# Attention scores in three blocks of 384 keys instead of two of 512 and one of 128, and a second buffer of output rows

## The chip, the cores and the metric

One core of a Trainium2 chip runs the whole program. The metric is the time of one execution on the device in microseconds (us). Below, TensorE is PE, VectorE is DVE, ScalarE is ACT, GpSimd is POOL, and SyncE, which issues most of the transfers, is SP.

## What is computed

Three layers follow each other: an attention, a mixture of experts that picks one expert per token, and a gated feed-forward layer. Only the attention is touched by the change. Its core is this, with batch 4, 8 heads, 1152 keys, heads of 64 and 576 queries (each the mean of two neighbouring rows of `q`):

```python
q_pool = q.reshape(B, H, S // 2, 2, D).mean(axis=3)
scores = np.matmul(q_pool, k.transpose(0, 1, 3, 2)) / np.sqrt(D)
scores = scores - np.max(scores, axis=-1, keepdims=True)
attn = np.exp(scores)
attn = attn / (np.sum(attn, axis=-1, keepdims=True) + 1e-09)
return np.matmul(attn, v)
# then: x = rows of tokens; moe picks e = argmax(x @ w_gate) and scales
#       relu(x @ w1[e]) @ w2[e]; last (silu(x @ w_gate) * (x @ w_val)) @ w_out
```

## The kernel before

The 32 heads are worked off in 16 pairs. In a pair each head has 576 queries: four tiles of 128 rows, and 64 rows that are left over. So a pair has nine tiles of query rows: tiles 0 to 3 of the first head, 4 to 7 of the second, and tile 8 with the left-over rows of both. For each tile a row of 1152 scores must be there before its maximum is known, and with it the exponentials.

All values are fp32; for precision the kernel splits operands into a high and a low part. A score tile is the sum of two matmuls (tile 8: of four) per block of keys. The row of 1152 keys was cut as 512 + 512 + 128:

- Two halves of 512 keys go to the PSUM banks `ps_s0` to `ps_s2`, taken in turn (`scores`, L785 to L792). Each half fills a bank.
- The last 128 keys of four tiles at once go to one further bank, `ps_r` (`scores_rem`, L805).
- DVE takes the maximum of each half (`largest_half`, L578) and, for four tiles at once, of the rests (`largest_rest`, L586), and then the negated maximum over the three (`neg_max`, L591).
- ACT computes the exponentials into `probs`, each with the sum of its row: `exp_half` (L538) and `exp_rem` (L521).
- PE turns the probabilities by 128x128 blocks into `ps_t` (`fill`, L694), ACT copies them to `p_hi` (L514), DVE takes the rest to `p_lo` (L657), and PE multiplies both with the values into `ps_o` (`products`, L761, and L770 for tile 8).
- The products of a head are copied out by DVE (`o_sb`, L598 and L601), PE turns them back (L725), and DVE scales them into the output rows `x_out` (L643, and L608 with L613 for tile 8). SP stores `x_out` to memory (`store`, L309 and L313).
- For the pair that follows, PE turns keys and queries in four groups (units "g"), ACT and DVE write high and low parts (`kept_rows`), and SP copies these to `kq_t`.

Three engines run the same list `UNITS` of 27 steps per pair, each in its own fixed order: "a" and "b" are the nine key chunks of the first and the second head, "c" tile 8 in three pieces, "g" the groups of the next pair, "x" the two turns of the results. "b" of one pair is worked off at the start of the body after it. At unit n PE fills one of the three buffers `ps_t` (which the unit three back must have left: `TR = 3`), and multiplies the unit three back (`LAG = 3`). The tables `SCORES_AT`, `MAXIMA_AT` and `EXP_AT` say behind which unit PE computes a tile's scores, DVE its maxima and ACT its exponentials; tile 0 in them is that of the next pair. A unit may have several of them. The first body ("first"), the last one ("last") and what is left after it ("tail") have only some of the units. Semaphores hold the engines to each other: `exp_done` says that a bank of scores is free, `t_free` that a `ps_t` is, `o_free` that `ps_o` is.

Of the kernel before, what the change touches and what calls it, by code (L numbers as in the profile page):

```python
# [8 lines left out]
ALU = mybir.AluOpType  # L9
# [3 lines left out]
P = 128  # L13
# [4 lines left out]
X_STORES = 3 * 16 + 1  # L18
# [4 lines left out]
class Shared:  # L23
# [3 lines left out]
    def __init__(self, nc, ctx, x_dram, experts, slot_tiles, ident, kept):  # L27
# [21 lines left out]
        self.x_out = sb("x_out", [P, 9 * 64])  # L49
        self.x_stored = ctx.enter_context(nc.semaphore("x_stored"))  # L50
# [11 lines left out]
def attention(nc, q, k, v, w_gate, w_out_gate, w1, x_dram, xs_dram, ys_dram, shared):  # L62
# [27 lines left out]
    MAIN = 8 * P  # L90
# [14 lines left out]
    SR = 3  # L105
# [9 lines left out]
    ]  # L115
    SCORES_AT = [(26, 26), (2, 2), (4, 5), (7, 8), (12, 13), (17, 17), (19, 20), (21, 22), (23, 24)]
    MAXIMA_AT = [(25, 25), (2, 2), (3, 4), (7, 8), (12, 13), (16, 16), (18, 19), (20, 21), (22, 23)]
    EXP_AT = [(0, 2, 2), (4, 4, 4), (7, 8, 8), (11, 11, 13), (16, 16, 17), (18, 19, 20), (21, 21, 21), (22, 23, 23), (25, 25, 25)]
# [3 lines left out]
    assert HALF_SCALE == 0.25 and len(UNITS) % TR == 0 and 2 * TILES % SR == 0  # L122
# [50 lines left out]
    with ctx:  # L173
# [21 lines left out]
        x_out, x_stored = shared.x_out, shared.x_stored  # L195
# [9 lines left out]

        S = [ps(f"ps_s{i}", 512) for i in range(SR)]
        R = ps("ps_r", 512)
# [15 lines left out]
        r_ready = sem("r_ready")  # L223
        max_done = sem("max_done")
        bias_ready = sem("bias_ready")
        exp_rem_done = sem("exp_rem_done")
# [16 lines left out]
        assert X_DMAS * PAIRS + 1 == X_STORES and x_out.shape[1] == TILES * D  # L243
# [25 lines left out]
        with nc.Block() as block:  # L269

            @block.sync
            def _(sp):
# [29 lines left out]
                def store(p, kind):  # L302
# [8 lines left out]
                        x_out[:, 0:QT * P].rearrange("p (t c) -> p t c", t=QT)).then_inc(x_stored, 16)  # L311
                    for h in range(2):
                        sp.dma_start(x_rows[bass.ds(b, 1), QT * P:SQ, bass.ds(g, 1), h * D:h * D + D].rearrange(  # L313
                            "b p g c -> (b p) (g c)"),
                            x_out[h * REM:h * REM + REM, QT * P:QT * P + D]).then_inc(x_stored, 16)
# [32 lines left out]
                zero_rows(0, 1).then_inc(x_stored, 16)  # L348
                with sp.Fori(1, LAST - 3, 2) as p:
                    next_pair(p, 1, "mid")  # L350
                    store(p - 1, "mid")
                    zero_rows(2 * p - 1, 2).then_inc(rows_zeroed, 16)
                    next_pair(p + 1, 0, "mid")
                    store(p, "mid")
# [5 lines left out]
                store(LAST - 3, "mid")  # L360
# [11 lines left out]
                store(LAST - 2, "mid")  # L372
# [3 lines left out]
                sp.wait_ge(x_stored, 16 * (X_DMAS * (LAST - 1) + 1))  # L376
# [4 lines left out]
                store(LAST - 1, "last")  # L381
                store(LAST, "tail")
# [107 lines left out]
            def _(act):  # L490
# [26 lines left out]
                def exp_rem(p, par, tile):  # L517

                    r = (tile % QT) * P
                    to = tile * SK  # L520
                    nc.scalar.activation(probs[:, to + MAIN:to + SK], R[:, r:r + P], ACT.Exp,  # L521
                                         bias=neg_max[:, tile:tile + 1],
                                         accum_out=sums[par][:, sum_col(tile, 2)]).then_inc(exp_rem_done, 1)

                def exp_half(p, par, kind, tile, h):

                    if h == 0:
# [7 lines left out]
                        if kind != "first" and tile == TC:  # L535
                            act.wait_ge(t_filled, upto(p, kind, every, UNIT_LAST["c"]))
                    at = tile * SK + h * 512
                    nc.scalar.activation(probs[:, at:at + 512], S[(2 * tile + h) % SR][:, :], ACT.Exp,  # L538
                                         bias=neg_max[:, tile:tile + 1],
                                         accum_out=sums[par][:, sum_col(tile, h)]).then_inc(exp_done, 1)  # L540

                def body(p, par, kind):
                    j = 0
                    for n, step in enumerate(UNITS):
# [3 lines left out]
                        for tile in range(TILES):  # L548
                            if kind != "tail" and EXP_AT[tile][0] == n:
                                exp_half(p, par, kind, tile, 0)  # L550
                            if kind != "tail" and EXP_AT[tile][1] == n:
                                exp_rem(p, par, tile)
                            if kind != "tail" and EXP_AT[tile][2] == n:
                                exp_half(p, par, kind, tile, 1)
# [7 lines left out]
            def _(dve):  # L562
# [18 lines left out]
                def largest_rest(p, tile):  # L581

                    if tile % QT == 0:
                        dve.wait_ge(r_ready, 3 * p + tile // QT + 1)
                        w = 1 if tile == TC else QT
                        nc.vector.tensor_reduce(  # L586
                            maxima[:, 3 * tile:3 * (tile + w)].rearrange("p (t s) -> p t s", s=3)[:, :, 2],
                            R[:, 0:w * P].rearrange("p (t c) -> p t c", t=w), AX, ALU.max).then_inc(max_done, 1)

# [70 lines left out]
                def body(p, par, kind):  # L660
                    j = 0
                    for n, step in enumerate(UNITS):
                        if step in steps(kind):
                            take(p, par, kind, j, step)
                            if lagged(kind, j) in UNIT_LAST.values():
                                outputs(p, kind, lagged(kind, j)[0])
# [1177 lines left out]
```

## Time and profile before

| | |
|---|---|
| median of three runs | 1478.25 us (1476.42 to 1483.18) |
| the profiled execution | 1476.28 us, of which its span is 1474.5 us |
| attention | from the start to some 607 us |
| one pair in its steady stage | 35.47 us |
| PE busy in that stage | 35.07 of 35.47 us |
| DVE busy | 32.82 of 35.47 us |
| ACT busy | 28.90 of 35.47 us |
| granted TensorE clock | full (2.4 GHz) all through that stage |

A matmul's busy time overlaps with that of the next one, so what a matmul costs is read from the distance of the starts, not from its duration. The same holds for DVE and ACT, where one instruction begins a little before the one ahead of it has ended.

### The profile page before, as it was taken

How to read it: one execution, taken by the hardware profiler on the slowest of the kernel's cores; microseconds unless marked ns; L12 is line 12 of the kernel's file. 1: busy time of each engine (PE TensorE's matmuls, PEld its weight loads, DVE VectorE, ACT ScalarE, POOL GpSimd, SP SyncE). 2: the span in 40 equal slices, each digit the busy share in tenths (PEclk: the TensorE clock that was granted, in tenths of full speed). 3: DMA queues.
4: the chain of work that ended last, by engine and by line, in shares of the span. 5: the costliest groups of instructions: out<-in, count | busy, mean ns of one | idle time of the engine just before them, and what ended most of it. 6: DMA issues, size and time to landing. Idle time of an engine off the chain costs nothing. (4 is left out here: it accounts for less than half of the span.)

```text
span 1474.5 us, 24891 instructions
## 1 busy us (share of the span) xinstructions
PE 1377.8 (93%) x7733; PEld 1195.3 (81%) x7734; DVE 873.2 (59%) x1658; ACT 638.4 (43%) x1549; POOL 345.2 (23%) x241
## 2 busy tenths in 40 slices
PE   3999999999999999739978999998999999999998
PEld 2788888888888888537767787887999999999997
DVE  2899999999999998673443444445632323223232
ACT  2888888788888887532034102004411111111111
POOL 3122222222222220279179205022101010100000
PEclk9999999999999999969998999999999999999999
DMA  7566666666666764356256313114400000000000
GB/s 164 124 139 139 138 138 142 146 144 145 145 149 145 195 132 153 101 193 247 88 199 233 116 43 107 43 57 142 150 32 15 29 15 17 26 0 21 0 22 22
DMA packets 127931, 156.85 MB, mean 106 GB/s; under 512 B 47633, under 2 KB 86545, under 8 KB 125841
## 3 DMA queue, kind: packets, MB, share of 16 engines
q1 hardware_dynamic: 111968, 114.35, 30.8%
q10 hardware_dynamic: 12880, 31.99, 6.5%
q0 software_dynamic: 3040, 9.96, 2.0%
q8 instruction: 25, 0.41, 0.1%
q14 instruction: 18, 0.14, 0.0%
HBM read 87.33 MB, written 29.10 MB: 79 GB/s over the span
## 5 line engine op out<-in xcount | busy, mean ns | idle before, releaser
L514 ACT ACTIVATE p_hi<-ps_t 128x512 fp32r<-128x512 f32 (+1 forms) x336 | 194.3, 586 | 69.1 <-PE ps_t L694 64.7
L657 DVE TENSOR_TENSOR p_lo<-ps_t,p_hi 128x512 fp32r<-128x512 f32 (+1 forms) x336 | 216.9, 666 | 12.4 <-ACT p_hi L514 7.8
L578 DVE TENSOR_REDUCE maxima<-ps_s 128x1 f32<-128x512 f32 x288 | 193.7, 686 | 41.5 <-PE ps_s L792 37.7
L538 ACT ACTIVATE probs<-ps_s,neg_max 128x512 f32<-128x512 f32 x288 | 198.6, 690 | 44.1 <-DVE neg_max L591 43.9
L792 PE MATMUL ps_s<-kq_t 128*128 128x512 f32 x640 | 199.7, 414 | 13.6 <-DMA kq_t<-kept_rows 9.5
L694 PE MATMUL ps_t<-ident,probs 128*128 128x128 f32 x1296 | 198.5, 274 | 1.4 <-DVE kept_rows L569 0.8
L1026 POOL TENSOR_TENSOR w_parts<-raw_w,w_parts 128x1024 fp32r<-128x1024 f32 x64 | 150.9, 2396 | 184.5 <-ACT w_parts L1096 184.4
L694 PEld LDWEIGHTS ps_t<-ident,probs 128*128 128x128 f32 x1296 | 156.0, 140 | 46.3 <-DVE p_lo L657 9.6
L1642 ACT ACTIVATE silu<-ps_g 128x384 f32<-128x384 f32 x72 | 35.4, 491 | 314.6 <-PE ps_g L1748 314.6
L1695 DVE TENSOR_TENSOR silu<-ps_g,silu 128x384 f32<-128x384 f32 x72 | 40.1, 558 | 210.7 <-ACT silu L1642 210.7
L1096 ACT ACTIVATE w_parts<-raw_w 128x1024 fp32r<-128x1024 f32 x64 | 67.1, 1059 | 220.0 <-PE ps_h L1423 104.2
L761 PE MATMUL ps_o<-p_hi,v_hl 128*128 128x512 f32 x288 | 137.7, 478 | 8.4 <-DVE o_sb L598 5.2
L792 PEld LDWEIGHTS ps_s<-kq_t 128*128 128x128 f32 x640 | 114.7, 192 | 37.9 <-DMA kq_t<-kept_rows 9.9
L761 PE MATMUL ps_o<-p_lo,v_hl 128*128 128x512 f32 x288 | 113.6, 394 | 0.0
L1746 PE MATMUL ps_g<-mxt_hi,wg 128*128 128x384 f32 x288 | 97.5, 339 | 2.4 <-DVE mxt_lo L1670 2.4
L1748 PE MATMUL ps_g<-mxt_hi,wg 128*128 128x384 f32 x288 | 97.7, 339 | 0.0
L1747 PE MATMUL ps_g<-mxt_lo,wg 128*128 128x384 f32 x288 | 97.2, 338 | 0.0
L1421 PE MATMUL ps_h<-w_parts,xst_hi 128*128 x200 | 83.0, 415 | 14.6 <-POOL w_parts L1026 11.9
L1748 PE MATMUL ps_v<-mxt_hi,wv 128*128 128x384 f32 x288 | 96.4, 335 | 0.0
L1746 PE MATMUL ps_v<-mxt_hi,wv 128*128 128x384 f32 x288 | 96.4, 335 | 0.0
L1747 PE MATMUL ps_v<-mxt_lo,wv 128*128 128x384 f32 x288 | 96.4, 335 | 0.0
L1446 PE MATMUL ps_y<-w_parts,ht_hi 128*128 x200 | 81.7, 409 | 5.4 <-DVE ht_lo L1289 2.8
(190 smaller groups left out, 2786.5 us busy)
## 6 DMA issues: line engine op xcount, KB each, us to landing
raw_w<-in_moe_w ACTq DMA_DIRECT2D x61, 512.0 KB, 4.1
kq_t<-kept_rows SPq DMA_DIRECT2D x32, 608.0 KB, 6.2
kq_t<-kept_rows SPq DMA_DIRECT2D x32, 320.0 KB, 7.1
raw_k<-in_k SPq DMA_DIRECT2D x32, 288.0 KB, 5.7
raw_v<-in_v SPq DMA_DIRECT2D x16, 576.0 KB, 5.5
kq_t<-kept_rows SPq DMA_DIRECT2D x32, 288.0 KB, 6.5
raw_q<-in_q SPq DMA_DIRECT2D x32, 256.0 KB, 4.1
y_by_slot<-x_out SPq DMA_DIRECT2D x25, 256.0 KB, 2.0
```

The lines of the kernel that those rows point to most:

```text
L514: nc.scalar.activation(p_hi[prob_ring(kind, m)][:, 0:w], T[ring(kind, j)][:, 0:w], ACT.Copy).then_inc(hi_ready, 1)
L538: nc.scalar.activation(probs[:, at:at + 512], S[(2 * tile + h) % SR][:, :], ACT.Exp, bias=neg_max[:, tile:tile + 1], accum_out=sums[par][: ...
L578: nc.vector.reduce_max(maxima[:, 3 * tile + h:3 * tile + h + 1], S[(2 * tile + h) % SR][:, :], AX).then_inc(max_done, 1)
L657: nc.vector.tensor_tensor(p_lo[n][:, 0:w], t[:, 0:w], p_hi[n][:, 0:w].bitcast(F32), ALU.subtract).then_inc(t_free, 1)
L694: last = nc.tensor.transpose(dst[:, n * P:(n + 1) * P], src, ident[:, :])
L761: last = nc.tensor.matmul(O[:, :], v_hl[v_par][:, c * P:(c + 1) * P], part[:, :], start=(i == 0 and n == 0), stop=(i == CH - 1 and n == 1))
L792: last = nc.tensor.matmul(S[(2 * tile + h) % SR][:, :], w, kq_t[par][:, at:at + 512], start=(n == 0), stop=(n == len(ops) - 1))
L1026: nc.gpsimd.tensor_tensor(w_part(n, parity, 1, at, PIECE), raw[j % RAW][:, :], w_part(n, parity, 0, at, PIECE).bitcast(F32), ALU.subtract) ...
L1421: nc.tensor.matmul(HB[h][:, :], xh, dyn(0, base, 0, at), start=(c == 0), stop=False)
L1746: nc.tensor.matmul(dst, wh, xh, start=(c == 0), stop=False)
L1747: nc.tensor.matmul(dst, wh, xl, start=False, stop=False)
L1748: last = nc.tensor.matmul(dst, wl, xh, start=False, stop=(c == DC - 1))
```

## The change

A score row is cut in three blocks of 384 keys. All blocks use the four PSUM banks that scores had together: block 0 goes to `ps_s0` and `ps_s3` in turn, block 1 always to `ps_s1`, block 2 to `ps_s2`. `ps_r`, its semaphores, `scores_rem`, `exp_rem` and `largest_rest` are gone. ACT takes the blocks of a tile in the order 1, 2, 0. The list `UNITS` and the tables of places have other entries (now three per tile). There are two buffers `x_out`, each with a semaphore of its own for its stores, and SP waits for both where it waited for one.

```diff
-    SCORES_AT = [(26, 26), (2, 2), (4, 5), (7, 8), (12, 13), (17, 17), ...
+    SCORES_AT = [(25, 26, 26), (2, 2, 2), (4, 5, 5), (6, 7, 7), (8, 12, 12), (12, 14, 15), ...
+    EXP_ORDER = (1, 2, 0)
...
-        S = [ps(f"ps_s{i}", 512) for i in range(SR)]
-        R = ps("ps_r", 512)
+        S = [ps(f"ps_s{i}", 512) for i in range(4)]
...
+        def bank(par, tile, b):
+            return S[b if b else 3 * ((par + tile) % 2)][:, 0:BLK]
...
-                    at = tile * SK + h * 512
-                    nc.scalar.activation(probs[:, at:at + 512], S[(2 * tile + h) % SR][:, :], ACT.Exp,
+                    at = tile * SK + b * BLK
+                    nc.scalar.activation(probs[:, at:at + BLK], bank(par, tile, b), ACT.Exp,
                                          bias=neg_max[:, tile:tile + 1],
-                                         accum_out=sums[par][:, sum_col(tile, h)]).then_inc(exp_done, 1)
+                                         accum_out=sums[par][:, sum_col(tile, b)]).then_inc(exp_done, 1)
...
-                def largest_half(p, tile, h):
-
-                    dve.wait_ge(s_ready, 2 * TILES * p + 2 * tile + h + 1)
-                    nc.vector.reduce_max(maxima[:, 3 * tile + h:3 * tile + h + 1],
-                                         S[(2 * tile + h) % SR][:, :], AX).then_inc(max_done, 1)
+                def largest(p, par, tile, b):
+
+                    dve.wait_ge(s_ready, 3 * (TILES * p + tile) + b + 1)
+                    nc.vector.reduce_max(maxima[:, 3 * tile + b:3 * tile + b + 1], bank(par, tile, b), AX
+                                         ).then_inc(max_done, 1)
+                    if b == 2:
+
+                        dve.wait_ge(max_done, 3 * (TILES * p + tile + 1))
+                        nc.vector.tensor_reduce(neg_max[:, tile:tile + 1], maxima[:, 3 * tile:3 * tile + 3], AX,
+                                                ALU.max, negate=True).then_inc(bias_ready, 1)
...
-                    dve.wait_ge(x_stored, 16 * (X_DMAS * (p - 1) + 1))
+                    dve.wait_ge(x_stored[1 - par], 8 * X_DMAS * (p - 1 - (1 - par)) + 16)
...
-                        pe.wait_ge(exp_done, 2 * TILES * p + 2 * tile + h - SR + 1)
+                        pe.wait_ge(exp_done, 3 * (TILES * p + tile - 1) + b)
...
-                        at = head * HEAD + h * 512
-                        last = nc.tensor.matmul(S[(2 * tile + h) % SR][:, :], w, kq_t[par][:, at:at + 512],
+                        at = head * HEAD + b * BLK
+                        last = nc.tensor.matmul(bank(par, tile, b), w, kq_t[par][:, at:at + BLK],
                                                 start=(n == 0), stop=(n == len(ops) - 1))
```

How the instructions stand now is seen best in the middle of a pair, where the last "b" products, the pieces of tile 8 ("c") and the groups of the next pair ("g") meet the scores of tile 4. First PE, before. `ps_t<-ident,probs` is a turn of probabilities (x3: a "c" piece), `ps_t<-ident,raw_k` one of keys (a "g" group), `ps_s` are scores of 512 keys, `ps_r` the rests of four tiles, ISA and REGISTER_ALU are waits and counters.

```order
L694 MATMUL ps_t<-ident,probs 128x128 x3
L785 REGISTER_ALU
L788 ISA
L792 MATMUL ps_s<-kq_t 128x512 x2
L706 REGISTER_ALU
L694 MATMUL ps_t<-ident,probs 128x128 x3
L785 REGISTER_ALU
L792 MATMUL ps_s<-kq_t 128x512 x2
L800 ISA
L805 MATMUL ps_r<-kq_t 128x128 x8
L706 REGISTER_ALU
L694 MATMUL ps_t<-ident,raw_k 128x128
```

And PE after the change; the scores here are blocks 1 and 2 of tile 4 and block 0 of tile 5, the products in rows 2 and 3 those of the last "b" chunk.

```order
L677 MATMUL ps_t<-ident,probs 128x128 x3
L744 MATMUL ps_o<-p_hi,v_hl 128x512
L744 MATMUL ps_o<-p_lo,v_hl 128x512
L677 MATMUL ps_t<-ident,raw_k 128x128 x4
L769 REGISTER_ALU
L776 MATMUL ps_s<-kq_t 128x384 x2
L769 REGISTER_ALU
L776 MATMUL ps_s<-kq_t 128x384 x2
L769 ISA
L776 MATMUL ps_s<-kq_t 128x384 x2
L689 REGISTER_ALU
L677 MATMUL ps_t<-ident,probs 128x128 x3
```

The eight matmuls on the rests are gone, the two score groups of 512 keys that stood one behind each "c" piece have become three of 384 in a row, and the group "g" 1, which stood ahead of the "c" pieces, now stands between the second and the third.

Then DVE at the same place, before: the copy of the second head's products (`o_sb`), the low parts of the "c" pieces, the maxima of both halves and of the rests, and the negated maximum.

```order
L601 COPY o_sb<-ps_o 128x512
L656 REGISTER_ALU
L657 TENSOR_TENSOR p_lo<-ps_t,p_hi 128x384
L577 REGISTER_ALU
L578 TENSOR_REDUCE maxima<-ps_s 128x1
L657 TENSOR_TENSOR p_lo<-ps_t,p_hi 128x384
L577 REGISTER_ALU
L578 TENSOR_REDUCE maxima<-ps_s 128x1
L584 ISA
L586 TENSOR_REDUCE maxima<-ps_r 128x4
L590 REGISTER_ALU
L591 TENSOR_REDUCE neg_max<-maxima 128x1
```

And DVE after the change.

```order
L643 TENSOR_TENSOR p_lo<-ps_t,p_hi 128x384
L587 COPY o_sb<-ps_o 128x512
L571 REGISTER_ALU
L572 TENSOR_REDUCE maxima<-ps_s 128x1
L571 REGISTER_ALU
L572 TENSOR_REDUCE maxima<-ps_s 128x1
L576 ISA
L577 TENSOR_REDUCE neg_max<-maxima 128x1
L571 REGISTER_ALU
L572 TENSOR_REDUCE maxima<-ps_s 128x1
L635 REGISTER_ALU
L563 SCALAR_TENSOR_TENSOR kept_rows<-ps_t,kept_rows 128x512
```

Behind the copy now stand two reductions of 384 (blocks 1 and 2 of tile 4), the negated maximum and block 0 of tile 5, with no low part between them; the low part of the third "c" piece comes after a `kept_rows`.

## Rows read from the trace of the kernel before

**Rows 1.** The page: the span, and the TensorE clock granted in 40 slices.

```profile
span 1474.5 us, 24891 instructions
...
PEclk9999999999999999969998999999999999999999
```

**Rows 2.** Busy us of PE, PEld, DVE, ACT, POOL; clock; DMA: thirteen pairs, one pair.

```profile
83.62:544.76 461.14, 455.97 (x2927) 387.97 (x2926) 427.03 (x872) 375.96 (x1028) 96.10 (x79) 1.00 0.63 146
331.92:367.39 35.47, 35.07 (x226) 29.85 (x225) 32.82 (x68) 28.90 (x80) 7.38 (x6) 1.00 0.63 143
```

**Rows 3.** Timeline of PE, one steady pair: start, duration, engine, line, what, [idle before].

```profile
340.05 1.09 PE L792 MATMUL ps_s<-kq_t 128*128 128x512 f32 x4
340.98 1.01 PE L805 MATMUL ps_r<-kq_t 128*128 128x128 f32 x8
341.82 0.62 PE L694 MATMUL ps_t<-ident,probs 128*128 128x128 f32 x4
342.20 0.48 PE L761 MATMUL ps_o<-p_hi,v_hl 128*128 128x512 f32 x1
```

**Rows 4.** Timeline of PE, last stage: its matmuls of 384 columns.

```profile
1154.69 0.33 PE L1746 MATMUL ps_g<-mxt_hi,wg 128*128 128x384 f32 x1
...
1158.87 0.39 PE L1761 MATMUL ps_out<-wo,a_hi 128*128 128x512 f32 x1
```

**Rows 5.** Timeline of PE, same pair: three places where it stands.

```profile
345.49 0.60 PE L694 MATMUL ps_t<-ident,probs 128*128 128x128 f32 x4
346.35 0.50 PE L761 MATMUL ps_o<-p_hi,v_hl 128*128 128x512 f32 x1 [0.26 <-DVE o_sb L598]
...
346.92 0.60 PE L694 MATMUL ps_t<-ident,probs 128*128 128x128 f32 x4
347.27 0.48 PE L761 MATMUL ps_o<-p_hi,v_hl 128*128 128x512 f32 x1
...
363.21 0.60 PE L694 MATMUL ps_t<-ident,probs 128*128 128x128 f32 x4
363.92 0.47 PE L761 MATMUL ps_o<-p_hi,v_hl 128*128 128x512 f32 x1
...
365.27 0.71 PE L792 MATMUL ps_s<-kq_t 128*128 128x512 f32 x2
365.98 0.66 PE L694 MATMUL ps_t<-ident,probs 128*128 128x128 f32 x4
```

**Rows 6.** Timeline of DVE, same pair: its reductions and what follows.

```profile
338.64 0.28 DVE L586 TENSOR_REDUCE maxima<-ps_r 128x1 f32<-128x128 f32 x1
...
340.71 1.29 DVE L578 TENSOR_REDUCE maxima<-ps_s 128x1 f32<-128x512 f32 x2 [0.41 <-PE ps_s L792]
342.02 0.69 DVE L586 TENSOR_REDUCE maxima<-ps_r 128x4 f32<-128x512 f32 x1
342.75 0.16 DVE L591 TENSOR_REDUCE neg_max<-maxima 128x1 f32<-128x3 f32 x1
...
358.03 0.55 DVE L657 TENSOR_TENSOR p_lo<-ps_t,p_hi 128x384 fp32r<-128x384 f32 x1
358.49 0.68 DVE L578 TENSOR_REDUCE maxima<-ps_s 128x1 f32<-128x512 f32 x1
```

**Rows 7.** Groups by form: busy us, mean ns, idle before: the exponentials on ACT.

```profile
L538 ACT ACTIVATE probs<-ps_s,neg_max 128x512 f32<-128x512 f32 x288 | 198.6, 690 | 44.1 <-DVE neg_max L591 43.9
...
L521 ACT ACTIVATE probs<-ps_r,neg_max 128x128 f32<-128x128 f32 x144 | 52.6, 365 | 0.0
```

**Rows 8.** Timeline of all engines, the opening: an exponential on ACT.

```profile
31.06 0.69 ACT L538 ACTIVATE probs<-ps_s,neg_max 128x512 f32<-128x512 f32 x1 [1.21 <-DVE neg_max L591]
```

**Rows 9.** Timeline of the SP queue, same pair: copies and stores.

```profile
363.86 2.59 SPq L299 DMA_DIRECT2D kq_t<-kept_rows  x1
...
380.79 1.33 SPq L313 DMA_DIRECT2D x_rows<-x_out  x2
```

**Rows 10.** The page, transfers: the copies of 320 KB, us to landing.

```profile
kq_t<-kept_rows SPq DMA_DIRECT2D x32, 320.0 KB, 7.1
```

More of the change, by code:

```diff
@@ L48, in __init__ @@
         self.raw_loaded = [ctx.enter_context(nc.semaphore(f"raw_w_loaded{i}")) for i in range(RAW)]
-        self.x_out = sb("x_out", [P, 9 * 64])
-        self.x_stored = ctx.enter_context(nc.semaphore("x_stored"))
+        self.x_out = sb("x_out1", [P, 9 * 64])
+        self.x_stored = [ctx.enter_context(nc.semaphore(f"x_stored{i}")) for i in range(2)]
         self.x_dram = x_dram
@@ L242, in attention @@
         KQ_DMAS, X_DMAS, COPIES = 6, 3, 3
[L243 removed]
+        assert X_DMAS * PAIRS // 2 + 1 == X_STORES and x_out[0].shape[1] == TILES * D
+        def bank(par, tile, b):
+            return S[b if b else 3 * ((par + tile) % 2)][:, 0:BLK]
         def sum_col(tile, part):
@@ L515, in take, with exps @@
                                          ).then_inc(hi_ready, 1)
[L517 to L527, printed above, removed]
+                def exps(p, par, kind, tile, b):
+                    if b == EXP_ORDER[0]:
                         act.wait_ge(bias_ready, TILES * p + tile + 1)
@@ L548, in body @@
                         for tile in range(TILES):
[L549 to L554, printed above, removed]
+                            for at, b in zip(EXP_AT[tile], EXP_ORDER):
+                                if kind != "tail" and at == n:
+                                    exps(p, par, kind, tile, b)
                 for g in range(GROUPS):
@@ L684, in _ @@
                     group_lo(g, g % TR)
-                largest_half(0, 0, 0)
-                largest_half(0, 0, 1)
-                largest_rest(0, 0)
+                for b in range(3):
+                    largest(0, 0, 0, b)
                 over_pairs(dve, body)
@@ L708, in fill @@
                     if what in "ab":
-                        done = 2 * TILES * p + (2 * QT if what == "a" else -2)
+                        done = 3 * (TILES * p + (QT if what == "a" else -1))
                         pe.wait_ge(exp_done, done)
@@ L779, in operands, with scores @@
                             for h in heads for part in range(2)]
-                def scores(p, par, tile, h, opening=False):
-                    if not (opening and 2 * tile + h < SR):
-                        pe.wait_ge(exp_done, 2 * TILES * p + 2 * tile + h - SR + 1)
-                    if tile in (0, QT) and h == 0:
+                def scores(p, par, tile, b, opening=False):
+                    if not (opening and (tile == 0 or (tile == 1 and b == 0))):
+                        pe.wait_ge(exp_done, 3 * (TILES * p + tile - 1) + b)
+                    if tile in (0, QT) and b == 0:
                         pe.wait_ge(kq_copied[tile // QT], 16 * COPIES * (p + 1))
@@ L822, in body @@
                             opening = kind == "first" and tile > 0
-                            if SCORES_AT[tile][0] == n:
-                                scores(*of, tile, 0, opening)
-                            if SCORES_AT[tile][1] == n:
-                                scores(*of, tile, 1, opening)
-                                if tile % QT == 0:
-                                    scores_rem(*of, tile, opening)
+                            for b in range(3):
+                                if SCORES_AT[tile][b] == n:
+                                    scores(*of, tile, b, opening)
                     if kind == "tail":
@@ L841, in _ @@
                     group(g, T[g % TR]).then_inc(t_filled, 1)
-                scores(0, 0, 0, 0, True)
-                scores(0, 0, 0, 1, True)
-                scores_rem(0, 0, 0, True)
+                for b in range(3):
+                    scores(0, 0, 0, b, True)
                 over_pairs(pe, body)
@@ L992, in _ @@
             def _(sp):
-                sp.wait_ge(shared.x_stored, 16 * X_STORES)
+                for i in range(2):
+                    sp.wait_ge(shared.x_stored[i], 16 * X_STORES)
                 for i in range(X_EARLY, len(X_LOADS)):
```

86 lines of the change are left out of this document (32 added, 54 removed), and 4 rows, old and new, of the table UNITS.

## The prediction

> **What bounds the kernel now.** I began with the page for the share of each engine and the granted clock. The clock is at its upper level (2.4 GHz) in nearly all slices of the attention [rows 1]; nothing in the change makes PE idle for long, so I price all of the steady stage at that level. Then I put the busy times of the engines side by side over thirteen pairs, each counted from the second turn of the results to the same turn of the next pair. The reader is to see that 461.14 / 13 = 35.47 us go to a pair, that PE is busy for 455.97 / 461.14 = 99% of it, DVE for 93% and ACT for 82% [rows 2]. So PE sets the pace, DVE is close behind (2.65 us free in a pair) and ACT is not in question.
>
> Busy time hides small stands of PE, since matmuls are pipelined. In the timeline I compared each group with the same group elsewhere. Four turns followed by products take 347.27 - 346.92 = 0.35 us from start to start; once in a pair they take 346.35 - 345.49 = 0.86, where the first products into `ps_o` wait for DVE's copy out of it, and once 363.92 - 363.21 = 0.71, where the same bank waits for tile 8's results [rows 5]. Two score matmuls, which by the price below take 0.465, take 365.98 - 365.27 = 0.71 before a turn that needs its `ps_t` [rows 5]. With three lesser ones that I found by the same comparison (some 0.3 together, an estimate) PE stands 0.50 + 0.36 + 0.25 + 0.3 = 1.4 us in a pair. Its own work is then 35.47 - 1.4 = 34.07.
>
> **The change on PE, which carries the forecast.** In a pair PE does 40 matmuls of 512 columns and 20 of 128 for scores: two parts by two halves for eight tiles, four by two for tile 8, and the rests likewise. Afterwards it is two parts by three blocks for eight tiles and four by three for tile 8, so 60 of 384. The count stays 60, and so do the columns (40 x 512 + 20 x 128 = 60 x 384 = 23,040). What changes is the price per matmul:
> - 512 columns: four take 340.98 - 340.05 = 0.93, or 0.2325 each [rows 3].
> - 128 columns: eight take 341.82 - 340.98 = 0.84, or 0.105 each [rows 3].
> - 384 columns: none in this stage, but the last stage runs 24 of them, with the same operand types, in 1158.87 - 1154.69 = 4.18, or 0.174 each [rows 4].
>
> The line through 384 and 512 would give a matmul of 128 columns 0.174 - 2 x 0.0585 = 0.057. It costs 0.105. These 20 short ones are what the change gets rid of: 40 x 0.2325 + 20 x 0.105 = 11.40 before, 60 x 0.174 = 10.44 after, 0.96 less in a pair. A group of turns right behind the short ones takes 342.20 - 341.82 = 0.38 [rows 3] instead of 0.35 [rows 5], three times in a pair, and the new order has one change fewer from turns to other matmuls (26 runs of turns in a pair against 27; each costs its successor some 0.08, by the same comparison of groups). Together 0.1 more. PE's own work becomes 34.07 - 1.06 = 33.0 us.
>
> The Trainium skill (TensorE: Matmul & The Clock Gate, section Back-to-back issue gap) says that in a stream of weight loads and matmuls the sustained spacing is some 81 ns at 128 columns and 131 ns at 512. By that the 60 matmuls cost 6.9 us before and, on the line between, 6.9 after: no gain at all. The trace does not agree (232.5 and 105 ns here), so I give it a small chance below.
>
> **DVE.** A reduction of 512 takes 0.68 to 0.69, one of 128 takes 0.28 [rows 6], so 384 should take 0.28 + 0.40 x 2/3 = 0.55, and being pipelined it holds the engine for about as long as the low part of 384 columns does, 358.49 - 358.03 = 0.46 [rows 6]. Two of 512 in a row last 1.29 together and one alone 0.69, so one holds it for 0.60 when something independent follows; it holds it for 0.73 when the negated maximum must wait for its end (342.75 - 342.02) [rows 6]. Per pair, before: 12 at 0.60, 6 at 0.73, 2 rests of four tiles at 0.73, one of 128 at 0.28 + 0.04: 13.4. After: 18 at 0.465 and 9 at 0.465 + 0.13 = 0.595: 13.7. The negated maxima stay. So DVE gets 0.3 to 0.4 us more, and needs 32.82 + 0.35 = 33.2 us of a pair if it never waits. That is a second floor, as high as PE's. It also caps the gain at 35.47 - 33.2 = 2.3 us a pair.
>
> The Trainium skill (VectorE: DVE Perf Modes, section on the TRN2 errata) warns that each instruction pays a fixed cost and advises tiles of 512 elements or more; with its 120 + N cycles for a PSUM source the reductions would cost 0.75 us more a pair instead of 0.35. The trace has a fixed part as well (0.28 for 128 against 0.68 for 512), and most of it is hidden by the instruction ahead.
>
> **ACT.** The exponentials take 690 ns for 512 and 365 ns for 128 [rows 7]; on that line 384 takes 365 + 325 x 2/3 = 582, and 3 x 582 = 1746 against 2 x 690 + 365 = 1745 per tile. Nothing changes, and each tile still has three.
>
> **Waits.** Blocks 1 and 2 now have one bank each. A tile's block 2 can be computed only when ACT is done with the last tile's blocks 1 and 2, and only then come its maximum, the negated maximum and the next exponentials. With nothing between, a round is two exponentials (1.15), two matmuls and their latency (0.35 + 0.3), a reduction (0.58) and the negated maximum (0.2): 2.6 us, nine rounds 23.4 of a pair of 34. So it has slack of a third, and the tables put one to two units (0.9 us each) between. I followed the new order unit by unit with the spacings above. The stand at the first copy of `ps_o` nearly goes: PE has six scores (1.04) ahead of it instead of four (0.93), and tile 0's maxima end some 0.4 earlier on DVE. A new one of some 0.3 arises behind the place shown for DVE, where the copy (0.60), three reductions and a negated maximum (1.7) and a `kept_rows` (0.65) stand before the buffer of "g" 1 is free; the wait for tile 8's results grows from 0.35 to about 0.5; single waits for an exponential give 0.2. That comes to 1.0 to 1.1. A count misses small latencies, and DVE has less room than before, so I take the old sum of 1.4. Bounds: 0.9 at the least (33.9 us a pair), and at the most what turns the gain round, below.
>
> **What stays at nothing.** The second `x_out` takes a wait from DVE that does not bind: the stores of the pair are issued from 380.79 to 382.1 [rows 9], and the next writer of `x_out` comes behind the "c" pieces, at 358.03 + 35.47 = 393.5 [rows 6]. SP's copies for the next pair come one unit earlier, and tile 0's scores one unit earlier too: the last copy for them is issued at 363.86 [rows 9] and lands 7.1 later [rows 10], at 371.0; its reader came at 340.05 + 35.47 = 375.5 [rows 3], and 3 us or so remain. In the opening, tiles follow each other bound by the round above (ACT stands 1.21 per tile for the negated maximum [rows 8]); a tile should take the same time, for one exponential more in the round (0.5) and shorter matmuls and reductions (0.25 and 0.15 less). I take 0, with -1.5 to +1.5.
>
> **The sum.** A pair takes 33.0 + 1.4 = 34.4 instead of 35.47, 1.07 less. It counts for the thirteen pairs of [rows 2], the one before and the one after them: 15 x 1.07 = 16 us. Nothing behind the attention changes. The profiled execution took 1476.3 and would take 1460; the median of the runs shown is 2 above it, and goes to 1462.
>
> **The rivals.**
> - *DVE takes over and eats the gain* (0.20). For it: DVE's floor of 33.2 is above PE's. Against: it still has 1.2 us free in a pair of 34.4. If it keeps most of its idle time (2.0 of 2.65), a pair takes 35.2 and the kernel 1474; with all of it 35.85 and 1484.
> - *Slower, by the single banks* (0.12). The round decides: if at each tile PE's turns and products fall between exponential and scores, so that a round costs 2.6 + 1.8 (two units) = 4.4 at half of the tiles and 3.5 at the others, a pair takes 35.5, and with a third unit at five tiles 37, 1.5 more: 1478 + 23 = 1501. It decides from 3.94 per round (35.47 / 9) on. Against it: block 0 has two banks and can be filled early, and the tables place exponentials ahead of the scores that need them.
> - *No gain on PE* (0.03). If 384 columns cost here 0.19 instead of 0.174, the 0.96 is gone and the kernel stays at 1478. Rows of 384 columns speak against it.
> - *More than forecast* (0.07). The stands fall to 0.9 or below: 15 x 1.6 = 24 less, 1454 or lower.
> - The forecast, 34.1 to 34.7 a pair, has the rest (0.58): 1457 to 1466.
>
> **How the numbers follow.** A difference of 0.5% (7 us) is about what a measurement can tell from none. Faster by more: 0.58 + 0.07 and a quarter of DVE's case, 0.70. Within: the rest of DVE's case and the one without gain, 0.18. Slower: 0.12. The range runs from 1453 to 1478 and leaves out the slower case and little below.
>
> **What would show it.** Right: a pair of about 34.4 in the timeline of PE, its score matmuls 0.174 apart, DVE's reductions 0.55 long and 27 in a pair, DVE's share at 96 to 97%, the 0.50 stand at the first copy mostly gone, the time behind the attention as before. Wrong: score matmuls further apart than 0.18, PE waiting in its scores for `probs` (the bank of ACT), or waits of PE for `p_lo` that come to more than 2 us a pair.

## The result and the profile after

The change makes the kernel slower: 1520.37 us (median of four runs, 1518.82 to 1521.09) against 1478.09 us for the kernel before in the same comparison, a ratio of 1.0273 with a 95% interval of 1.0253 to 1.0292. The forecast was 1462 us and its range ended at 1478, so it has the wrong sign. Each ratio below is likewise against runs of the kernel before that were made beside the runs of the edit (medians 1480.12, 1482.87 and 1481.55 us).

The page of the changed kernel answers to [rows 1]: the span is 44.8 us longer, and the mean granted clock is down to 0.8 in two slices of the attention, where it was 0.9 or more before. The last row counts the packets of a queue that fetches instructions; on the page of the kernel before it had 18 packets and 0.14 MB.

```profile
span 1519.3 us, 25250 instructions
...
PEclk9998989999999999995998999999999999999999
...
q14 instruction: 48, 0.39, 0.1%
```

The windows answer to [rows 2]; columns as there. The first is the opening up to the second turn of the results, the second the thirteen pairs behind it, the third the rest. The last two are neighbouring pairs.

```profile
0.00:82.38 82.38, 56.47 (x302) 48.09 (x304) 49.12 (x108) 45.74 (x127) 21.44 (x29) 1.00 0.60 134
82.38:590.95 508.57, 465.06 (x2926) 407.69 (x2926) 429.98 (x950) 371.11 (x1028) 95.65 (x79) 0.95 0.58 133
590.95:1519.30 928.35, 863.52 (x4508) 764.33 (x4507) 397.99 (x698) 216.43 (x396) 227.39 (x135) 0.97 0.26 84
162.18:196.84 34.66, 34.46 (x227) 30.56 (x227) 33.07 (x74) 28.56 (x80) 7.41 (x7) 1.00 0.62 147
196.84:241.44 44.60, 37.56 (x227) 32.52 (x227) 33.11 (x74) 28.64 (x80) 7.32 (x7) 0.89 0.50 115
```

The thirteen pairs take 508.57 instead of 461.14, 47.4 more; the opening takes 1.2 less and all that follows 1.4 less (928.35 against 1474.5 - 544.76 = 929.74). So the whole loss lies in the steady stage, and there in every second pair. Counted from second turn to second turn the pairs last 34.67, 45.13, 34.66, 44.60, 34.66, 44.21, 34.68, 44.04, 34.66, 43.99, 34.68, 43.90, 34.69. Seven are short, 0.80 below the 35.47 of before; six are long, by 9.64 above the short ones on the mean. 6 x 9.64 - 13 x 0.80 = 47.4: the sum closes.

The long ones have a hole on DVE. This is DVE's timeline around the first of them (start, duration, engine, line, what; in brackets the idle time before it and what ended it).

```profile
126.67 1.64 DVE L572 TENSOR_REDUCE maxima<-ps_s 128x1 f32<-128x384 f32 x3
128.34 0.16 DVE L577 TENSOR_REDUCE neg_max<-maxima 128x1 f32<-128x3 f32 x1
128.44 0.69 DVE L643 TENSOR_TENSOR p_lo<-ps_t,p_hi 128x512 fp32r<-128x512 f32 x1
137.30 1.89 DVE L643 TENSOR_TENSOR p_lo<-ps_t,p_hi 128x512 fp32r<-128x512 f32 x3 [8.17 <-issue]
```

DVE ends its work at 129.1 and starts the next instruction at 137.3. It isn't kept by another engine: "issue" says that it waited for nothing that the profile shows. When it comes back it does three low parts in a row that had piled up. The place is always the same. DVE's fixed order runs in a loop whose body (`over_pairs`, L265) is two pairs long, the first "mid" body with parity 1 and the second with parity 0, and the hole is where the end of that body meets its beginning. Seven rounds have six jumps back, and there are six holes. The waits of the attention (engine, line, what for: us in total, times, longest) show who hangs on them:

```profile
ACT p_hi L519 <- PE ps_t L677: 102.3, 121, 7.5
DVE p_lo L643 <- issue: 49.3, 6, 8.3
...
PE ps_t L677 <- DVE p_lo L643: 36.4, 6, 6.1
```

PE's timeline at the same place:

```profile
130.40 1.64 PE L776 MATMUL ps_s<-kq_t 128*128 128x384 f32 x6
138.05 1.11 PE L677 MATMUL ps_t<-ident,probs 128*128 128x128 f32 x4 [6.00 <-DVE p_lo L643]
139.84 0.80 PE L744 MATMUL ps_o<-p_hi,v_hl 128*128 128x512 f32 x1 [0.68 <-DVE o_sb L584]
...
143.21 1.05 PE L677 MATMUL ps_t<-ident,probs 128*128 128x128 f32 x4
143.91 0.78 PE L744 MATMUL ps_o<-p_hi,v_hl 128*128 128x512 f32 x1
```

PE's next turns need a `ps_t` that DVE has not left (`t_free`), so PE stands for 6.0 us and then for another 0.68. The granted clock fell while PE stood, and PE resumes at the lower level (1.2 GHz): four turns take 143.91 - 143.21 = 0.70 from start to start where they take 0.35 in [rows 5]. The windows show the clock (the number before the last two) at 0.50 and then back at 1.00:

```profile
135.30:138.00 2.70, 0.00 (x0) 0.00 (x0) 0.70 (x2) 0.00 (x0) 0.59 (x2) 0.50 0.52 188
138.05:145.50 7.45, 6.77 (x22) 5.60 (x23) 5.17 (x10) 3.48 (x9) 0.00 (x0) 0.50 0.00 1
145.60:150.00 4.40, 4.40 (x29) 3.89 (x28) 4.18 (x10) 3.21 (x9) 0.00 (x0) 1.00 0.00 0
```

In the pair from 196.84 the mean granted clock is 0.89, and 9.94 us are lost on a hole of some 8: the hole is paid once as waiting and then again in slow matmuls.

Where there is no hole, the kernel does about what the prediction said. PE in the short pair:

```profile
163.88 0.60 PE L677 MATMUL ps_t<-ident,probs 128*128 128x128 f32 x4
164.54 0.61 PE L776 MATMUL ps_s<-kq_t 128*128 128x384 f32 x2
...
168.29 1.55 PE L776 MATMUL ps_s<-kq_t 128*128 128x384 f32 x8
169.69 0.60 PE L677 MATMUL ps_t<-ident,probs 128*128 128x128 f32 x4
...
175.34 1.64 PE L776 MATMUL ps_s<-kq_t 128*128 128x384 f32 x6
176.81 0.60 PE L677 MATMUL ps_t<-ident,probs 128*128 128x128 f32 x4
```

Eight score matmuls take 169.69 - 168.29 = 1.40, or 0.175 each. Two stands are to be seen: 164.54 - 163.88 = 0.66 for four turns, 0.31 over their 0.35, and 176.81 - 175.34 = 1.47 for six scores, 0.42 over 6 x 0.175. PE's weight loads (PEld) name the cause of both, a bank of scores that ACT has not left:

```profile
164.54 0.30 PEld L776 LDWEIGHTS ps_s<-kq_t 128*128 128x128 f32 x2 [0.30 <-ACT probs L535]
...
176.36 0.30 PEld L776 LDWEIGHTS ps_s<-kq_t 128*128 128x128 f32 x2 [0.47 <-ACT probs L535]
```

And from the page, the reductions and the exponentials of 384:

```profile
L535 ACT ACTIVATE probs<-ps_s,neg_max 128x384 f32<-128x384 f32 x432 | 247.8, 580 | 52.3 <-DVE neg_max L577 52.3
...
L572 DVE TENSOR_REDUCE maxima<-ps_s 128x1 f32<-128x384 f32 x432 | 228.7, 550 | 34.9 <-PE ps_s L776 28.4
```

### The profile page after: what moved, and what is told of

Its sections match the earlier page's. It is cut to its first block and busy times, and to the rows that moved or that the text cites. A ratio compares the mean times of both kernels' runs of the same rounds, so it can differ in the third digit from the quotient of the medians.

```text
span 1519.3 us, 25250 instructions
## 1 busy us (share of the span) xinstructions
PE 1385.1 (91%) x7733; PEld 1220.1 (80%) x7734; DVE 877.1 (58%) x1754; ACT 633.3 (42%) x1549; POOL 344.5 (23%) x241
## 5 line engine op out<-in xcount | busy, mean ns | idle before, releaser
L535 ACT ACTIVATE probs<-ps_s,neg_max 128x384 f32<-128x384 f32 x432 | 247.8, 580 | 52.3 <-DVE neg_max L577 52.3
L776 PE MATMUL ps_s<-kq_t 128*128 128x384 f32 x960 | 237.0, 360 | 17.5 <-DMA kq_t<-kept_rows 9.4
L572 DVE TENSOR_REDUCE maxima<-ps_s 128x1 f32<-128x384 f32 x432 | 228.7, 550 | 34.9 <-PE ps_s L776 28.4
L677 PE MATMUL ps_t<-ident,probs 128*128 128x128 f32 x1296 | 203.3, 279 | 36.9 <-DVE p_lo L643 36.8
L677 PEld LDWEIGHTS ps_t<-ident,probs 128*128 128x128 f32 x1296 | 165.5, 144 | 61.9 <-DVE p_lo L643 39.3
L776 PEld LDWEIGHTS ps_s<-kq_t 128*128 128x128 f32 x960 | 170.5, 195 | 53.3 <-ACT probs L535 20.9
L1610 ACT ACTIVATE silu<-ps_g 128x384 f32<-128x384 f32 x72 | 35.4, 492 | 313.9 <-PE ps_g L1716 313.9
L744 PE MATMUL ps_o<-p_hi,v_hl 128*128 128x512 f32 x288 | 141.6, 492 | 6.7 <-DVE o_sb L584 5.2
L744 PE MATMUL ps_o<-p_lo,v_hl 128*128 128x512 f32 x288 | 116.7, 405 | 0.0
L409 POOL TENSOR_TENSOR v_hl<-raw_v,zeros 128x1152 fp32r<-128x1152 f32 x16 | 42.3, 2647 | 236.2 <-PE ps_o L753 236.0
```

The costliest lines, as they stand in the source:

```text
L535: nc.scalar.activation(probs[:, at:at + BLK], bank(par, tile, b), ACT.Exp, bias=neg_max[:, tile:tile + 1], accum_out=sums[par][:, sum_col( ...
L572: nc.vector.reduce_max(maxima[:, 3 * tile + b:3 * tile + b + 1], bank(par, tile, b), AX).then_inc(max_done, 1)
L677: last = nc.tensor.transpose(dst[:, n * P:(n + 1) * P], src, ident[:, :])
L744: last = nc.tensor.matmul(O[:, :], v_hl[v_par][:, c * P:(c + 1) * P], part[:, :], start=(i == 0 and n == 0), stop=(i == CH - 1 and n == 1))
L776: last = nc.tensor.matmul(bank(par, tile, b), w, kq_t[par][:, at:at + BLK], start=(n == 0), stop=(n == len(ops) - 1))
```

## The experiments

The theory that the two traces suggest: DVE's loop body has grown by the split of the rows (nine tiles with three reductions each instead of two, two pairs in a body, and a counter or wait for most of them; the four-tile rests are gone), and no longer stays in what DVE keeps of its code, so that each jump back has to fetch it. The trace records 249 of DVE's instructions per round before and 282 after: 12 reductions and 21 counters and waits more. The expectations below count 281, one less, which changes none of what follows from it. The rivals: the second buffer of output rows, and the banks with their new order.

**The loop alone.** DVE's bodies are written out one after the other, with nothing else changed, so that DVE never jumps back.

```diff
-                over_pairs(dve, body)
+                body(0, 0, "first")
+                for q in range(1, LAST, 2):
+                    body(q, 1, "mid")
+                    body(q + 1, 0, "mid")
+                # then "last" and "tail" as before
```

> The changed kernel with DVE's loop over the pairs written out: the same DVE work in the same order, but as one straight line of instructions with no jump back and no register arithmetic for the waits. In the changed kernel every second pair takes 44 to 45 us instead of 34.67, and in each of these DVE stands 8.2 us right behind the end of its loop body, with nothing released that it waits for. Theory F (fetch): DVE's instructions are no longer at hand when it jumps back. Then the six stands of 8.2 us go, every pair takes about 34.6 us, and the kernel takes 1520 - 6 x 9.5 = 1463 us. Theory W (waits): the stand comes from the order of the work (the alternating bank of block 0 or the alternating output buffer, which also have a period of two pairs). Then it stays, and the kernel takes 1515 to 1520.

Measured: 1466.93 us, ratio 0.9914 (0.9886 to 0.9942). No stand on DVE for issue above 0.3 us is left in the steady stage, and the pairs take 34.5 and 34.7 in turn. DVE does the same work in the same order; the jump and the register arithmetic for the waits have gone, and 53 us with them. The next runs part the two.

**The same loop at another place.** The loop is kept, and an argument of it sets at which instruction, counted within the blocks of code, DVE's body begins.

```diff
-            with eng.Fori(1, LAST, 2) as p:
+            with nc.Fori(1, LAST, 2, engines=[eng.engine],
+                         head_slot={mybir.EngineType.DVE: 0}) as p:
```

> The changed kernel, with the first instruction of DVE's loop body placed at the start (slot 0) of a block of 256 instructions; the loop and all work are as they were. Theory F in its form by position (the body must lie in two such blocks; 281 instructions from slot 0 do): the stands go, 1463 us. Theory F in its form by length (a body of more than 256 instructions never stays, 249 before did and 281 does not): nothing changes, 1520. Theory W: 1520.

Measured: 1470.96 us, ratio 0.9939 (0.9912 to 0.9966); the stands went as expected, but the kernel is 8 us above the 1463 expected. Its thirteen pairs (columns as above) and its instruction packets:

```profile
85.22:537.69 452.47, 449.23 (x2926) 397.13 (x2926) 429.98 (x950) 371.22 (x1028) 95.82 (x79) 1.00 0.64 149
```

```profile
q14 instruction: 19, 0.16, 0.0%
```

With 236 in place of the 0:

> As the run before, but the body starts at slot 236, so that its 281 instructions end in a third block (236 + 281 = 517). Theory F by position: the stands are there as in the changed kernel, 1515 to 1525 us. By length: 1520. Theory W: 1520. It tells something only together with the run before.

Measured: 1504.27 us, ratio 1.0174 (1.0149 to 1.02). The pair with the jump takes 40.4 to 41.4, and the stand is there again, but at 4.6 us instead of 8.2, so that the kernel stays below the 1515 to 1525 expected:

```profile
DVE p_lo L644 <- issue: 27.5, 6, 4.6
```

```profile
q14 instruction: 49, 0.40, 0.1%
```

One kernel, with nothing but its place in the code moved, is 33 us slower or faster, with the jump and all its arithmetic in both. What is fetched is seen as well: 30 packets more, five for each of the six jumps. They come round by round: in the changed kernel two fall into the stand from 208.9 to 217.1 and three into the rest of that round, while the kernel before has not one between 140 and 555 us.

**One buffer of output rows**, everything else as changed.

```diff
-        x_out, x_stored = [sb("x_out0", [P, TILES * D]), shared.x_out], shared.x_stored
+        x_out, x_stored = [shared.x_out, shared.x_out], shared.x_stored
...
-                    dve.wait_ge(x_stored[1 - par], 8 * X_DMAS * (p - 1 - (1 - par)) + 16)
+                    if not (isinstance(p, int) and p == 1):
+                        dve.wait_ge(x_stored[par], 8 * X_DMAS * (p - par) + 16)
```

> The changed kernel with a single buffer of output rows again (its two semaphores and the loop kept; DVE waits for the stores of the pair before). Theory F: the loop body has 282 instructions instead of 281, the stands stay, 1520 us. Theory W with the alternating output buffer as its cause: every pair is like the other, near 34.7 us, and the kernel near 1465.

Measured: 1528.06 us, ratio 1.0331 (1.0298 to 1.0364). The six stands are there (49.5 us in total), the short pairs take 34.76. The second buffer is not what costs. Without it the kernel is rather some 0.6% slower still, of which 0.1 us is seen in each short pair; 4.7 of the 6.3 us between the two spans lie behind the thirteen pairs, a stretch that takes 928 to 937 us in the fourteen traces whatever was changed. The prediction had put this buffer at nothing.

**How much is held.** Two more places, 228 and 108.

> The changed kernel with DVE's loop body at slot 228, eight slots ahead of the run at 236: its 281 instructions then end at 228 + 281 = 509 and lie in two blocks of 256. Theory F by position (two blocks are held): no stands, near the run at slot 0 (1471 us). If what counts is something finer (blocks of 128, or the place of the loop's end), the stands are there: 1500 us or more.

Measured at 228: 1470.61 us, ratio 0.992 (0.9903 to 0.9937), 18 packets, no stand.

> The changed kernel with DVE's body at slot 108: 108 + 281 = 389, two blocks of 256, but four of 128 (0 to 127 up to 384 to 511). At slots 0 and 228 it lay in three blocks of 128, at 236 in four. If what is held are blocks of 256, two of them: no stands, 1471 us. If it is three blocks of 128: stands, 1500 us or more.

Measured at 108: 1505.55 us, ratio 1.0165 (1.0133 to 1.0198):

```profile
DVE p_lo L644 <- issue: 27.2, 6, 4.6
```

```profile
q14 instruction: 50, 0.41, 0.1%
```

A packet is 8 KB (0.41 MB in 50). The Trainium skill (Runtime: NRT & Kernel Launch, section Instruction fetch mechanics) says that 256 instructions are 16 KiB, by which a packet would be 128 instructions (an estimate). Counted in blocks of 128, the body of 282 lies in three from 0 (to 282) and from 228 (to 510, blocks 128 to 511), and in four from 236 (to 518) and from 108 (to 390). In blocks of 256 it lies in two from 0, 228 and 108 and in three from 236. Only the first count sorts the four times rightly: three blocks of 128 without a stand, four with one. The Trainium skill's two lines of 256 would have spared the body at 108, and it isn't spared. By the same count a body of 249 can never lie in more than three, wherever it begins (127 + 249 = 376, under 384), and one of 282 lies in four if it begins at 103 to 127 of a block (236 and 108 are both at 108 of one). That the old body of 249 is spared everywhere is this count's word; the old kernel was not run with its start at 236 and nothing else changed.

**Why 8.2 us at one place and 4.6 at the others.** DVE's register instructions are in the trace too, and they show that the changed kernel waits twice. The first instruction of the body (a register operation of L265) comes 4.5 to 4.7 us after the jump, and the second another 4.0 to 4.1 after it, at each of the six jumps. At 236 and 108 there is one wait of 4.9 to 5.1, and the second instruction follows within 0.1; at 0 and 228 the first comes after 0.2 to 0.3. So in the changed kernel the first instruction seems to lie alone at the end of its block (slot 127 of 128), and the next is in a block that must be fetched as well. From 127 the body reaches 409, which is four blocks, as the count asks. The run with one output buffer has the same pair of waits.

**The old kernel with a body of the new length.** 32 memsets of one element each (0.06 us each) are added to DVE's body, which makes 249 + 32 = 281 instructions (282 in the trace, with a register move), and the body begins at 236. Blocks, banks, tables and buffer are those of before.

```diff
+        spare = sb("spare", [P, 32])
...
+                    if kind == "mid" and what in "ab":
+                        if i < 8:
+                            k = 16 * par + 8 * (what == "b") + i
+                            nc.vector.memset(spare[0:1, k:k + 1], 0.0)
```

> The kernel before with 32 tiny writes of one element in DVE's loop (16 a pair), so that its body has 281 instructions like the changed one, and with the body at slot 236. Scores, order and buffers are those of before. Theory F: six stands on DVE at the loop's end as in the changed kernel at slot 236, some 5.9 us a loop; with 1 us a pair at the most for the writes the kernel takes 1478 + 36 + 0 to 15 = 1514 to 1529 us. Theory W (the new order or the new banks): no stands, 1478 to 1493.

Measured: 1522.37 us, ratio 1.0273 (1.0252 to 1.0294): the kernel before loses 40 us with none of the change in it. That the ratio is the changed kernel's own is chance: it has the shorter stands (4.6 against 8.2 us) and not the gain of the short pairs. Two neighbouring pairs, the wait and the packets:

```profile
162.32:197.79 35.47, 35.08 (x227) 29.83 (x225) 32.96 (x84) 28.89 (x80) 7.38 (x6) 1.00 0.62 143
197.79:240.36 42.57, 38.00 (x227) 31.88 (x225) 33.02 (x84) 29.02 (x80) 7.37 (x6) 0.92 0.53 120
```

```profile
DVE spare L642 <- issue: 26.8, 6, 4.7
```

```profile
q14 instruction: 48, 0.39, 0.1%
```

The pair without the jump is at the old 35.47 to the hundredth, so the memsets themselves cost nothing. The pairs with it take 41.2 to 42.8. Length and start were changed together here.

And the kernel before with DVE's bodies written out (the edit of the first experiment):

> The kernel before with DVE's loop written out, as in the first run for the changed one. It had no stands at the loop's end, so the gain is only that of the register arithmetic of the waits: 0 to 5 us, 1474 to 1480. If the score blocks are what makes the changed one faster when it is written out (35.47 against 34.6 a pair), this stays some 12 us above it.

Measured: 1480.27 us, ratio 0.9976 (0.996 to 0.9991), pairs of 35.18. The kernel before loses nothing like this at its jumps. Against the changed kernel written out in the same way (0.9914, pairs of 34.5 and 34.7) it stays 0.6% above: that is what the change gains where no jump is in the way.

**A hint at the jump.** The loop is told to announce its jump back, on DVE; first with the body where the changed kernel has it, then at 236.

```diff
+            with nc.Fori(1, LAST, 2, engines=[eng.engine], hint_back_edge=True) as p:
```

Measured: 1470.84 us, ratio 0.9923 (0.9905 to 0.9941); 18 packets.

> The changed kernel with DVE's body at slot 236, where it had stands of 4.6 us, and with the hint that names the jump. The hint at the old place left only 18 packets on the queue for instructions, as if nothing had been fetched anew. If the hint makes DVE keep or fetch in time what it needs, no stands: 1471 us, and the packets tell which (18: kept, some 48: fetched ahead). If the hint only shifted the body to a good place there, the stands of the run at 236 are back: 1504.

Measured: 1469.81 us, ratio 0.9908 (0.9877 to 0.9938); 20 packets, pairs of 34.67 and 34.96, no stand. The hint mends both places. But it does so in a way that I did not expect: I had thought that the blocks would still be fetched, only in time, with 48 packets. They aren't fetched again, and that at 236 too, where the body lies in four blocks. So what is held cannot be simply "three blocks and no more"; the place and the hint both decide it. One reading would fit every count here: there is room for four blocks, and without a hint DVE also fetches the block behind the one that it is in, so that a body in four blocks needs a fifth (five packets in each round), one in three needs four (none), and the hint puts the jump's target in place of the block behind (none). No run tests this reading, and how the hint works stays open.

**The blocks without the new order.** Blocks of 384, their banks and both buffers, with the list `UNITS` and the places of before (blocks 1 and 2 where the second half stood or next to it), DVE's body at 0.

> Blocks of 384 keys, four banks and two output buffers as in the changed kernel, DVE's loop body at slot 0, but the units and the places of scores, maxima and exponentials as in the kernel before (block 0 where the first half stood, block 1 where the second stood or with it, block 2 with the second). It parts the price of the matmuls from the order. If the price is what gains: PE's own work in a pair is again 33.1 us, and with stands of 1.6 to 2.2 a pair takes 34.7 to 35.3, the kernel 1470 to 1479. If the order is what gains, a pair takes 35.4 or more, the kernel 1480 or more.

Measured: 1494.89 us, ratio 1.0087 (1.0057 to 1.0118). The second of the two cases expected came true (35.4 or more, 1480 or more). With these banks the price of the matmuls alone brings no gain, as thirteen pairs show, and the waits for the banks:

```profile
88.50:559.44 470.94, 457.11 (x2927) 394.70 (x2927) 434.69 (x950) 375.62 (x1028) 96.27 (x85) 1.00 0.62 143
```

```profile
PEld ps_s L777 <- ACT probs L536: 24.1, 52, 0.8
...
PE ps_s L777 <- ACT probs L536: 7.7, 20, 0.5
```

A pair takes 36.23, 0.75 more than before. Four times in each of thirteen pairs PE's weight load waits for ACT to be done with a bank of scores; with the new order and the body at 0 the row over its thirteen pairs reads `11.0, 33, 0.5`. So the new order is worth 470.94 - 452.47 = 18.5 us in thirteen pairs, 1.42 a pair, and is what makes the single banks bearable.

**The fastest.** DVE's and ACT's bodies both written out, the edit of the first experiment twice.

> The changed kernel with the loops of DVE and ACT written out, the candidate for the fastest. A pair took 34.51 and 34.70 us in turn with DVE's alone. ACT is busy for some 29 us of it, so its register arithmetic can cost only where PE waits for an exponential: 0 to 0.2 us a pair less, 1464 to 1467 where the first run had 1467.

Measured: 1462.49 us, ratio 0.9864 (0.9837 to 0.9891): this version is faster than both kernels, by 1.4% against the kernel before.

```profile
80.93:526.59 445.66, 444.08 (x2927) 398.18 (x2927) 425.32 (x950) 370.41 (x1028) 95.85 (x79) 1.00 0.65 152
```

A pair takes 34.28 (445.66 / 13), 1.19 less than before. That is 0.33 less than with DVE's loop alone written out (450.00 / 13 = 34.62), where 0 to 0.2 was expected. ACT's jump and its register arithmetic are worth that together; they were not parted.

## Why the prediction was wrong

**The step that failed** is its first paragraph: "nothing in the change makes PE idle for long, so I price all of the steady stage at that level", and with it the part on DVE, which counted what the reductions last ("DVE gets 0.3 to 0.4 us more") and never how many instructions the body of the loop has. That number went from 249 to 282, and the body began where 282 instructions don't stay. What the runs showed in place of a PE that never idles: DVE stands 8.2 us behind each of six jumps, PE stands 6.0 of them and then works on at 1.2 GHz. The same kernel with the body at 0 takes 452.47 us for the thirteen pairs instead of 508.57, so the stands cost 56.1 us, which no term of the sum and none of the rivals held. The one slower rival had another mechanism, and the range left it out. Undoing the stands in five ways (written out, two places, a hint at the own place and at 236) gives ratios of 0.991 to 0.994, and bringing length and place into the kernel before gives 1.0273. The growth alone does not cost (starts at 0 and 228): it takes the length and the start together.

The Trainium skill (Runtime: NRT & Kernel Launch, section Instruction fetch mechanics) warns that a taken branch whose target lies outside a window of two pages stalls the engine until the page is there. The trace agrees that there is such a stall, 8.2 us for each jump of the changed kernel. It could have been a rival, with the instructions counted in the two programs. It would not have been a firm one: the Trainium skill gives no price for it, and its window of 512 instructions holds 282 as well as 249, unless the body begins badly.

**PE's own work** was right: 0.174 per matmul of 384 columns forecast, 0.175 measured, in place of 0.2325 and 0.105. The doubt from the Trainium skill's spacing figures was rightly given little: the 60 matmuls of 384 take 60 x 0.175 = 10.5 us here, not the 6.9 estimated from them. One addition in the term is loose: 3 x 0.03 for the turns behind the short matmuls and 0.08 for the change fewer make 0.17, where 0.1 was taken.

**The stands** were mis-sized. I took 1.4 us a pair; the short pair takes 34.66, so the 33.0 of work forecast leave 1.65 (1.7 with the 0.17 above), where the count by hand had said 1.0 to 1.1. The stand of 0.50 at the first copy of `ps_o` has gone, as forecast. But where I had put 0.2 for single waits for an exponential there are 0.31 and 0.42, at the two places shown above: the single banks took back the larger part of what that stand had cost. The short pair gained 0.80 instead of 1.07.

**Every second pair** takes 0.3 more than the other even where nothing is fetched (34.67 and 34.96 with the body at 228 or at 0), while all pairs of the kernel before take 35.45 to 35.50. With that the mean gain is 0.66 a pair, 8.7 us in thirteen (461.14 - 452.47), and the kernel comes to some 1471 us rather than 1462. DVE's jump is the lesser part of it: with its loop written out 0.2 is left (34.5 and 34.7), and with ACT's written out too it is still 0.13 to 0.21. The bank of block 0 and the output buffer alternate from pair to pair as well; neither was tried in a kernel without stands, so the cause of the rest stays open.

**DVE and ACT.** 550 and 580 ns per block, forecast 0.55 us and 582 ns. DVE is busy for 33.07 of a short pair (forecast 33.2 of 34.4): it did not take over.

**The single banks** were a rival at 0.12, with 35.5 to 37 us a pair. With the old order it came out at 36.23. With the new one and the body at 0, PE's weight loads wait 11.0 us for them in thirteen pairs, 0.85 a pair. The rival's mechanism is real and the tables hold it off. Its upper price was too low by its own terms: a third unit of 0.9 us at five tiles adds 4.5 us to 35.5, not 1.5.

**The opening and the rest**: -1.2 us (forecast 0, with 1.5 either way) and -1.4, the latter well within what this stretch differs by from trace to trace (928 to 937 us). **The second buffer** was put at nothing, and is worth 0.1 us in a short pair.

## What to carry to other kernels

Where an engine's work runs in a loop, count the instructions of the body on each engine, counters and waits included, before and after a change, as one counts bytes for a buffer: past the point at which the code is held, every round pays microseconds, however little the added instructions last (shown here for DVE). Whether it pays depends on where the body begins, so an edit ahead of a loop can also bring or take such a stand; six "issue" stands at one line and more packets on the instruction queue are its mark. And a stand on an engine off the critical path is priced with the slow matmuls that follow it.

## What the hardware showed that I had not expected

- A jump back cost DVE 8.2 us for each round in the changed kernel and 4.6 us with the body at 236 or at 108, with the same 30 packets more. The first is two waits, of 4.6 us before the body's first instruction and of 4.1 before its second; the other is one.
- Without a hint a body that lies in three blocks of 8 KB by the count above fetched nothing at its jumps, and one in four was fetched anew in every round (four places and one padded body); with a hint nothing was fetched again at either place tried.
- After a stand of 6 us PE ran at 1.2 GHz from 138.05 to 145.5. The groups from there to 145.90 take 7.85 us; at the starts of full clock they would take 3.75 (a turn group 0.35, a pair of products 0.55, a score matmul 0.175). By this estimate some 3.0 us go to the clock and 1.1 to the wait for `o_sb`.
